# Attention and mixer on one core: the load queue without its waits on earlier landings

## What is computed

```python
def _attn_ref(q, k, v):
    block, window = (32, 16)
    nb = S // block
    k_sum = k.reshape(B, H, nb, block, D).max(axis=3)
    v_sum = v.reshape(B, H, nb, block, D).mean(axis=3)
    scores_l = scale * np.matmul(q, k.transpose(0, 1, 3, 2))
    mask_l = np.abs(pos[:, None] - pos[None, :]) < window
    scores_s = scale * np.einsum('bhsd,bhnd->bhsn', q, k_sum) + np.log(block)
    scores_all = np.concatenate([np.where(mask_l, scores_l, -1e9), scores_s], axis=-1)
    a = softmax(scores_all)
    return np.matmul(a, np.concatenate([v, v_sum], axis=2))

def _moe_ref(x, w_in, w_spatial, b_spatial, w_out):        # 512 -> 1024 -> 512
    h = np.maximum(x @ w_in, 0.0)
    u, v = h[..., :512], h[..., 512:]
    v_n = (v - mean(v)) / np.sqrt(var(v) + 1e-06)
    v_s = np.einsum('ts,bsd->btd', w_spatial, v_n) + b_spatial[None, :, None]
    return (u * v_s) @ w_out

def _moe2_ref(x, w_in, conv_w, w_out):                     # 512 -> 1024 -> 512
    h = np.maximum(x @ w_in, 0.0)
    gate = sigmoid(conv over the tokens, 3 taps, of h)
    return (h * gate) @ w_out
```

## Time and profile before

| | |
|---|---|
| median of 3 runs | 345.57 us (345.17 to 345.75) |
| the profiled execution | 345.75 us, of which the span is 344.0 us |
| TensorE (PE) busy | 334.8 us, 97% of the span |
| VectorE (DVE) busy | 211.6 us, 62% |
| ScalarE (ACT) busy | 123.3 us, 36% |
| GpSimd (POOL) busy | 117.5 us, 34% |
| DMA | 24.72 MB in the span |

### The profile page before, as it was taken

How to read it: one execution, slowest core, us unless ns; L and a number is a source line. 1 busy time by engine, 2 the same in 40 slices (tenths; PEclk the granted TensorE clock), 3 DMA queues, 4 the chain that set the end, 5 groups by cost and what they waited for, 6 DMA issues and landing times.

```text
span 344.0 us, 7123 instructions
## 1 busy us (share of the span) xinstructions
PE 334.8 (97%) x2886; PEld 301.1 (88%) x2886; DVE 211.6 (62%) x503; ACT 123.3 (36%) x364; POOL 117.5 (34%) x130
## 2 busy tenths in 40 slices
PE   6899899999999999999999999999999999999995
PEld 6787788789998899889999999999999999999984
DVE  5688686352149960663447975787666667755552
ACT  3678788655241332541111124212222233222212
POOL 7568697756449999100007900000000000000000
PEclk9999999999999999999999999999999999999999
DMA  7777887100404200371002000000000004000004
GB/s 250 202 241 232 257 252 243 56 2 3 124 0 115 85 0 2 99 216 54 0 0 52 11 2 1 0 2 0 0 2 0 0 32 152 0 2 0 1 2 184
DMA packets 9026, 24.72 MB, mean 72 GB/s; under 512 B 1185, under 2 KB 1185, under 8 KB 8993
## 3 DMA queue, kind: packets, MB, share of 16 engines
q1 hardware_dynamic: 8992, 24.26, 22.8%
HBM read 21.11 MB, written 3.15 MB: 71 GB/s over the span
## 4 chain that ended last, share of the span: by engine, by line
PE 87%; DMA 10%; SPq 1%; DVE 0%; issue 0%; DVEq 0%
PE bank L807 27%; PE bank L809 26%; PE bank L808 26%; DMA qT<-in_q 4%; PE bank L799 3%; DMA kT<-in_k 3%; DMA vw<-in_vw 3%; PE bank L786 2%; PE bank L766 2%; PE bank L857 1%; PE bank L776 1%; DMA out<-obuf 1%; PE bank L860 0%; SPq L282 0%; DVE obuf L710 0%; SPq L271 0%
## 5 line engine op out<-in xcount | busy, mean ns | idle before, releaser
L809 PE MATMUL bank<-g_h,W_l 128*128 128x384 f32 x128 | 43.0, 336 | 0.0
L808 PE MATMUL bank<-g_l,W_h 128*128 128x384 f32 x128 | 42.9, 336 | 0.0
L807 PE MATMUL bank<-g_h,W_h 128*128 128x384 f32 x128 | 42.9, 335 | 0.0
L513 ACT ACTIVATE P<-P,nmax 128x120 f32<-128x120 f32 x96 | 36.7, 384 | 15.0 <-DVE nmax L642 15.0
L809 PE MATMUL bank<-wo_h,hg_l 128*128 128x512 f32 x96 | 38.0, 396 | 0.0
L808 PE MATMUL bank<-wo_l,hg_h 128*128 128x512 f32 x96 | 38.0, 396 | 0.0
L807 PE MATMUL bank<-wo_h,hg_h 128*128 128x512 f32 x96 | 37.9, 395 | 0.0
L809 PE MATMUL bank<-wsT_h,vn_l 128*128 128x384 f32 x96 | 32.1, 334 | 0.0
L807 PE MATMUL bank<-wsT_h,vn_h 128*128 128x384 f32 x96 | 32.1, 334 | 0.0
L808 PE MATMUL bank<-wsT_l,vn_h 128*128 128x384 f32 x96 | 32.1, 334 | 0.0
L570 ACT ACTIVATE cbuf<-cbuf 128x768 f32<-128x768 f32 x16 | 13.5, 846 | 49.5 <-DVE cbuf L724 49.5
(11 more groups left out here) (111 smaller groups left out, 791.6 us busy)
## 6 DMA issues: line engine op xcount, KB each, us to landing
vw<-in_vw SPq DMA_DIRECT2D x16, 288.0 KB, 4.4
kT<-in_k SPq DMA_DIRECT2D x8, 384.0 KB, 5.5
qT<-in_q SPq DMA_DIRECT2D x8, 384.0 KB, 4.0
out<-obuf SPq DMA_DIRECT2D x12, 256.0 KB, 2.4
stage<-in_wsT SPq DMA_DIRECT2D x6, 384.0 KB, 3.1
stage<-in_w SPq DMA_DIRECT2D x4, 512.0 KB, 3.7
stage<-in_wo SPq DMA_DIRECT2D x4, 512.0 KB, 3.6
wi_most<-in_w_in SPq DMA_DIRECT2D x3, 512.0 KB, 5.9
```

Source lines behind the costliest of these rows:

```text
L513: a.activation(P[:, i % NP_, j, :], P[:, i % NP_, j, :], ACT.Exp, bias=nmax[:, c:c + 1], scale=-1.0, accum_out=rsum[:, c, 0:1]).then_inc(e ...
L807: t_.matmul(dst, lhs[0](c), rhs[0](c), start=first, stop=False)
L808: t_.matmul(dst, lhs[0](c), rhs[1](c), start=False, stop=False)
L809: ins = t_.matmul(dst, lhs[1](c), rhs[0](c), start=False, stop=last)
```

## The change

All waits in SP's loop on landings of earlier transfers go. The waits on free buffers inside the three helpers stay, and so does the order of the issues.

```diff
             for p in range(NP):
-                if p >= 2:
-                    sp.wait_ge(q_in[(p - 1) % NQB], 16 * ((p - 1) // NQB + 1))
                 load_k(p)
-                if p >= 2:
-                    sp.wait_ge(v_in[(p - 1) % NVB], 32 * ((p - 1) // NVB + 1))
                 load_q(p)
-                if p >= 2:
-                    sp.wait_ge(k_in[p % NQB], 16 * (p // NQB + 1))
                 load_v(p)
                 if 2 <= p < 2 + KC:
-                    sp.wait_ge(q_in[p % NQB], 16 * (p // NQB + 1))
                     load_wi(p - 2)
```

## The result

The changed kernel takes 349.83 us (median of 4 runs, 348.58 to 351.9), the kernel before took 345.37 us beside it (4 runs, 343.43 to 345.75). The ratio is 1.0116, with a 95% interval of 1.0068 to 1.0166: the change makes the kernel slower by 1.2%. A second measurement (7 runs) gave 1.0103 (1.0072 to 1.0133). I had forecast 344.4 us. The profiled execution took 350.21 us, with a span of 348.3 us against 344.0 before.

The account below looks back on a forecast made before the run. PE was taken as the bound, fully busy from 36.72 us, with at most 2.2 us to gain from loads. 345.75 - 1.21 (slot 11) - 0.07 (slot 5) = 344.47, by the median 344.29; forecast 344.4 us, range 343.8 to 345.7.

Parts of the forecast that it names:

- Slot 11's wait for values goes: Slot 11, values of pair 4: issued near 22 us, the 1.14 us wait goes, 1.21 us gained in all.
- Instruction fetches ... I take 0: PE's pauses without releaser, perhaps from instruction packets: bounds -0.54 to +1.16 us, taken as 0 because the load queue is already busy.
- The rule that a delay of PE before 36.72 reaches the end: PE is busy from 36.72 to 338.00 us, so an earlier delay, or its removal, reaches the end unshortened.
- The second one: Denser transfers bring PE pauses by instruction packets, +1.16 us, eating the gain: 345.6 us; chance 0.11.
- The first one, a lagging DMA engine: An engine losing its catch-up pauses lands pair 4's values 4.5 us late for slot 11: 349.1 us; chance 0.09.

Follow-up runs that it names:

- e6: The kernel before with as many landing waits, but values issued before queries in each turn: 346.6 us, ratio 1.0033 (12 runs).
- e8: The kernel before with as many landing waits, but values issued before queries from pair 2 on only: 344.94 us, ratio 0.9992 (12 runs).
- e4: The changed kernel with all its landing waits put back for turns p = 4 to 7 only: 347.88 us, ratio 1.0068 against the kernel before (10 runs).
- e1: The changed kernel with 18 warm-up transposes on PE instead of 15: 349.02 us, one run, beside 345.44 for the kernel before.
- e3: The changed kernel with all its landing waits put back for turns p = 2 and 3 only: 348.43 us, ratio 1.0102 against the kernel before (10 runs).
- e5: The kernel before, landing waits kept, plus three unused loads of 512 KB after the values of pair 6: 345.63 us, ratio 1.000 (10 runs).
- e12: The kernel before, landing waits kept, plus three unused loads of 64 KB after the values of pair 6: 344.36 us, one run, beside 344.30.
- e9: The changed kernel with keys and queries of pairs 3 to 7 loaded for 192 of 768 positions only: 348.89 us, ratio 1.0109 (2 runs).
- e10: The changed kernel measured again, unchanged: 348.58 us, ratio 1.0103 against the kernel before.

## Why the prediction was wrong

- **Slot 11's wait for values goes: right.** The values of pair 4 were issued at 23.90 us (I had near 22), and PE did not wait for them. That issue is later than forecast because it waits for the values of group 2 (L791 at 23.18 for 0.69), which stand behind the first pause. The 1.14 us were real as a wait; the gain was lost to a pause of 1.81 us at the border after 717 matmuls, in the same slot. Little of that pause lay under the wait of before: there the packet started at 33.59 us, so by the 2.35 to 2.98 us of the other pauses the block was there at about 35.9 to 36.6, and without the wait PE would have come to the border at 36.3 (37.51 less 1.21). In e6 and e8, where the queue is paced, slot 11 has neither the wait nor a pause. I had checked what is late next among semaphores only (maxima, products, copies), and all of those were in time.
- **"Instruction fetches ... I take 0": this step failed.** The rows had shown both signs, two pauses with no releaser in the fastest slots and a queue of instruction packets, and I had set +1.16 us as the upper bound. The sum of pauses went from 0.57 to 3.91 us, +3.34, with two pauses and not five. The reason I gave for 0, that the packets met a busy queue already, confused the share of time in which the engines are busy with the length of what is queued: about two loads outstanding before, some 2.6 MB after (6.55 MB issued by 14.9 us, less 308 GB/s over the 12.9 us from 2.0).
- **The fall of the clock was not in the prediction at all.** It is worth 1.5 us behind the first pause (e4 against the changed kernel). Behind the second, slot 12 took 3.98 us instead of 2.84, another 1.1. Up to slot 13 the sum of the changed kernel is: 2.10 - 0.34 = +1.76 pause, +1.48 clock (5.01 us to slot 7 against 3.53), -0.17 earlier start, -0.50 in slot 9 (0.23 of it its pause), +0.99 in slot 11 (the pause and a slow start against the wait of before), +1.14 clock in slot 12, together 4.70. PE keeps these to its end (the last L801 at 344.57 against the last L809 at 339.85, 4.72). The span is only 4.3 us longer, because what follows PE and VectorE's last copy, the store of the result, took 0.4 us less in this execution.
- **The rule that a delay of PE before 36.72 reaches the end: right**, in the direction I had not forecast, as the 4.70 us at slot 13 and the 4.72 at PE's end show.
- **Rivals.** The second one (the gain is eaten by pauses of PE by instruction packets) named the mechanism, with 0.11 and too small a price. The first one, a lagging DMA engine, did not happen: no PE wait for loads after slot 0. I had quoted a rule of the Trainium skill (DMA: Bandwidth & Descriptors, "Queues, rings and completion order"), that a DMA engine goes round its queues packet by packet, as one that makes a long backlog harmless to a fetch. The packets came 1.5 and 3.7 us later behind a full queue (18.67 against 20.15; 49.29 against 53.01), so as I used it, it does not hold here.

What is shown is that the pause belongs to the instruction stream (e1, and the counts of matmuls in all profiles), that a long load queue makes it large (e3 and e4, and e5 against e12), and that the packet comes later with it. That bytes are the measure of that queue is not shown (e9). Where in the DMA path the packet loses the time was not tried.

## What to carry to other kernels

Idle time of an engine with no releaser, in a group of instructions that has no semaphore in it, is a sign of instructions that have not come. Count the matmuls between two such gaps, and if the numbers are multiples of one, ask what else uses the DMA engines then. A wait on an earlier load that seems to do nothing but delay can be what keeps the queue short enough for the instruction packets. And before a wait is counted as a gain, look at what else can come late once it is gone, instruction packets included, and at what a pause of TensorE does to its clock.

## What the runs showed of the hardware that I had not expected

- A pause of PE of 1.8 to 2.3 us can be followed by a stretch at the 1.2 GHz level (0.57 of full over 24 to 28 us) or not (e4 and e10: 2.09 us and full clock). Both happened.
- In light slots PE used a block of about 124 matmuls in some 5 us (247 in the 10.5 us between its two pauses before). A pause ended 2.35 to 2.98 us after the packet's start in all 22 cases, and the kernel before was already at the edge of what the fetches could follow (0.34 and 0.23 us of pause with two loads outstanding). After 60 us, where matmuls come fewer to the microsecond, no such pause stands in any profile.
- The first loads, whose issue no kernel here changes except e6, land at different times from one execution to the next: the fill of slot 0 started at 7.79 to 9.09 us. Later landings vary too (slot 11's wait 0.79 to 1.78 us with the same code up to there).
